# Softmax totals inverted by chunk and applied to x1 where the networks load it

## The reference, cut to what matters

```python
# attention: B=2, C=128, 12288 queries and 768 keys per batch
kv_pool = kv.reshape(B, H//4, 4, W//4, 4, C).mean(axis=(2, 4))
k = v = kv_pool.reshape(B, -1, C) @ w_sr
s = (q @ k.transpose(0, 2, 1)) / np.sqrt(C)
s = s - s.max(-1, keepdims=True)
a = np.exp(s)
a /= a.sum(-1, keepdims=True) + 1e-09
x1 = (a @ v).reshape(B * N, C)
# first network, d_ff = 2048
h = x1 @ moe_w_in
x2 = (h * np.cos(h)) @ moe_w_out
# second network
h = x2 @ moe2_w_in
out = (h / (1 + np.exp(-1.702 * h))) @ moe2_w_out
```

## Time and profile before

| | |
|---|---|
| median of 3 runs | 2651.97 us |
| span of the profiled execution, first to last instruction | 2650.0 us |
| PE busy | 2642.2 us (100%) |
| DVE busy | 2174.3 us (82%) |
| ACT busy | 1929.0 us (73%) |
| POOL busy | 2038.4 us (77%) |
| attention, joining stretch, networks | to about 554 us, to about 600 us, to 2650.0 us |

### The profile page before, as it was taken

The page is one execution under the profiler, slowest core; times in us unless marked ns, Lnnn a source line. Parts: engine busy times, 40 slices in busy tenths (PEclk is TensorE's granted clock), DMA queues, the critical chain, the costliest instruction groups (busy, mean ns, idle before and its releaser), DMA issues.

```text
span 2650.0 us, 40918 instructions
## 1 busy us (share of the span) xinstructions
PE 2642.2 (100%) x12551; PEld 2213.6 (84%) x12551; DVE 2174.3 (82%) x2786; ACT 1929.0 (73%) x2502; POOL 2038.4 (77%) x1900
## 2 busy tenths in 40 slices
PE   9999999999999999999999999999999999999999
PEld 8888888888888888888888888888888888888887
DVE  8999899987778787878787878787888888787876
ACT  5777777787777777777777777777777777777776
POOL 4887677579787878888878787878887878787873
PEclk9999999999999999999999999999999999999999
DMA  7323222200000000000000000000000000000000
GB/s 204 72 48 97 61 48 48 52 21 13 8 16 8 16 9 15 15 9 16 8 16 8 16 8 16 8 16 8 16 8 16 8 16 8 16 8 16 11 10 13
DMA packets 217397, 67.66 MB, mean 26 GB/s; under 512 B 200336, under 2 KB 201488, under 8 KB 216336
## 3 DMA queue, kind: packets, MB, share of 16 engines
q1 hardware_dynamic: 216304, 67.07, 11.0%
q10 hardware_dynamic: 1056, 0.13, 0.0%
HBM read 42.01 MB, written 25.17 MB: 25 GB/s over the span
## 4 chain that ended last, share of the span: by engine, by line
PE 99%; DVE 0%; DMA 0%; ACT 0%; SPq 0%; issue 0%
PE psum L644 29%; PE psum L645 29%; PE psum L646 29%; PE psum L691 7%; PE psum L848 5%; DMA kv_all<-in_kv 0%; PE psum L746 0%; DVE kv_all L1136 0%; DVE g_lo L1308 0%; PE psum L728 0%; PE psum L762 0%; PE psum L661 0%; DVE kv_all L1139 0%; PE psum L668 0%; ACT g_hi L1078 0%; PE psum L735 0%
## 5 line engine op out<-in xcount | busy, mean ns | idle before, releaser
L629 POOL TENSOR_TENSOR g_lo<-g,g_hi 128x512 fp32r<-128x512 f32 x768 | 1132.8, 1475 | 62.3 <-ACT g_hi L1085 2.2
L1308 DVE TENSOR_TENSOR g_lo<-g,g_hi 128x1024 fp32r<-128x1024 f32 (+1 forms) x396 | 666.8, 1685 | 413.9 <-ACT g L1080 413.9
L1078 ACT ACTIVATE g_hi<-psum 128x1024 fp32r<-128x1024 f32 (+1 forms) x396 | 397.3, 1003 | 557.3 <-PE psum L646 557.3
L626 POOL CAST g_hi<-g 128x512 fp32r<-128x512 f32 x750 | 503.8, 672 | 341.7 <-DVE g L1299 341.7
L644 PE MATMUL psum<-x_hi,w_lo 128*128 128x512 f32 x1536 | 597.9, 389 | 0.0
L644 PE MATMUL psum<-g_hi,w_lo 128*128 128x512 f32 x1536 | 597.7, 389 | 0.1
L646 PE MATMUL psum<-x_hi,w_hi 128*128 128x512 f32 x1536 | 597.6, 389 | 0.0
L645 PE MATMUL psum<-x_lo,w_hi 128*128 128x512 f32 x1536 | 597.5, 389 | 0.0
L646 PE MATMUL psum<-g_hi,w_hi 128*128 128x512 f32 x1536 | 597.5, 389 | 0.0
L645 PE MATMUL psum<-g_lo,w_hi 128*128 128x512 f32 x1536 | 597.5, 389 | 0.0
L1299 DVE TENSOR_TENSOR g<-psum,g 128x512 f32<-128x512 f32 x768 | 489.7, 676 | 1.9 <-ACT g L1071 1.8
(11 more groups left out here) (104 smaller groups left out, 2779.0 us busy)
## 6 DMA issues: line engine op xcount, KB each, us to landing
x_dram<-x_out SPq DMA_DIRECT2D x48, 256.0 KB, 2.0
x_raw<-x_dram SPq DMA_DIRECT2D x48, 256.0 KB, 2.7
out<-y_blocks SPq DMA_DIRECT2D x190, 64.0 KB, 2.3
q_blocks<-in_q SPq DMA_DIRECT2D x184, 64.0 KB, 2.2
kv_all<-in_kv SPq DMA_DIRECT2D x6, 1024.0 KB, 9.7
kv_all<-in_kv SPq DMA_DIRECT2D x4, 1536.0 KB, 12.0
w_raw<-in_moe_w_in SPq DMA_DIRECT2D x2, 1024.0 KB, 4.9
q_blocks<-in_q SPq DMA_DIRECT2D x2, 256.0 KB, 5.1
```

Of the source, the lines that this page charges most:

```text
L626: nc.gpsimd.tensor_copy(g1_hi[at][:, t], g1[at][:, t]).then_inc(g1_hi_ready, 1)
L629: nc.gpsimd.tensor_tensor(g1_lo[at][:, t], g1[at][:, t], g1_hi[at][:, t].bitcast(F32), ALU.subtract).then_inc(g1_lo_ready, 1)
L1078: nc.scalar.activation(g2_hi[ring2(j, p)][:, t], h2[buffer2(j)][:, t], ACT.Silu, scale=GELU)
L1308: nc.vector.tensor_tensor(g2_lo[ring2(j, p)][:, t], g2[ring2(j, p)][:, t], g2_hi[ring2(j, p)][:, t].bitcast(F32), ALU.subtract).then_inc(g ...
```

## The change

`scale` on POOL, `invert_total` on DVE and the one scaling of the first subtile on DVE go. The exponentials write their totals into eight columns, two chunks of four. Once a chunk, at the third subtile, DVE adds 1e-9 to four totals and inverts them (`invert_totals`), and SP saves the four columns to `inverse_dram` (`save_inverse`), 512 numbers of four bytes that go from 128 partitions to token order. PE waits for `exp_done` where it waited for `probs_ready`. x1 is stored unnormalised. `load_x1` issues a second DMA, which copies the chunk's 512 inverses to all 128 partitions (`x1_inv`), and `round_x1` on POOL multiplies x1 by them before it rounds it. POOL's remaining work in the attention is no longer tied to steps: folds, `unscale_piece` and `split_piece` run one behind another as soon as their data is there, the splits after `values_summed` has reached 24.

```diff
+            def save_inverse(c, n):
+                sp.wait_ge(inverse_ready, c + 1)
+                sp.dma_start(inverse_dram[c].rearrange("(j p) -> p j", p=P),
+                             inverse[:, n * SUB:(n + 1) * SUB],
+                             allow_slow_non_contiguous=True).then_inc(inverse_saved[n], 16)
...
             def load_x1(c, n):
                 sp.dma_start(x1_raw[n][:, :], x1_dram[c]).then_inc(x1_loaded[n], 16)
+                sp.dma_start(x1_inv[n][:, :],
+                             inverse_dram[c].rearrange("(o n) -> o n", o=1).to_broadcast([P, TOK])
+                             ).then_inc(x1_loaded[n], 16)
...
             with sp.Fori(0, 6) as r:
                 for n in range(2):
                     load_queries(r * 2 + (n + 10), n)
+                    save_inverse(r * 2 + (n + 7), 1 - n)
                     save_x1(r * 2 + (n + 5), 1 - n)
...
             for c in range(2):
                 sp.wait_ge(x1_saved[c], 16)
+                sp.wait_ge(inverse_saved[c], 16)
                 load_x1(c, c)
             for c in range(CHUNKS - 5, CHUNKS):
                 save_x1(c, c % 2)
+                if c + 2 < CHUNKS:
+                    save_inverse(c + 2, c % 2)
...
             def round_x1(c, n, loads):
-                pool.wait_ge(x1_loaded[n], 16 * loads)
+                pool.wait_ge(x1_loaded[n], 32 * loads)
+                nc.gpsimd.tensor_tensor(x1_raw[n][:, :], x1_raw[n][:, :], x1_inv[n][:, :],
+                                        ALU.mult).then_inc(x1_scaled, 1)
+                pool.wait_ge(x1_scaled, c + 1)
                 pool.sem_inc(x1_taken, 1)
                 nc.gpsimd.tensor_copy(x1_hi[n][:, :], x1_raw[n][:, :]).then_inc(x1_hi_ready, 1)
...
-            for s in range(FIRST_SPLIT):
-                if s > 0:
-                    scale(s, s % ROUND)
-                if s == SUB + 1:
-                    lower_queries(0)
...
+            lower_queries(0)
+            for s in range(UNITS * FOLDS):
+                fold(*divmod(s, FOLDS))
+            pool.wait_ge(unscale_made, 1)
+            pool.wait_ge(raw_loaded[3], 16)
+            for m in range(F // WP_COLS):
+                unscale_piece(m)
...
+            pool.wait_ge(values_summed, CB)
+            with pool.Fori(0, WEIGHT_PIECES // SUB) as r:
+                for p in range(2 * SUB):
+                    split_piece(r * SUB + p // 2, p % 2)
+            for c in range(2):
+                round_x1(c, c, 1)
...
-                    pe.wait_ge(probs_ready, s + (b * SB + 1))
+                    pe.wait_ge(exp_done, s + (b * SB + 1))
...
+            def invert_totals(c, n, saves):
+                cols = slice(n * SUB, (n + 1) * SUB)
+                dve.wait_ge(exp_done, c * SUB + SUB)
+                nc.vector.tensor_scalar(total[:, cols], total[:, cols], 1e-9, None,
                                         ALU.add).then_inc(total_guarded, 1)
+                if saves is not None:
+                    dve.wait_ge(inverse_saved[n], saves * 16)
+                dve.wait_ge(total_guarded, c + 1)
+                nc.vector.reciprocal(inverse[:, cols], total[:, cols]).then_inc(inverse_ready, 1)
...
-            invert_total(0, 0)
-            dve.wait_ge(inverse_ready, 1)
-            nc.vector.tensor_scalar(probs[0][:, :], probs[0][:, :], inverse[:, 0:1], None,
-                                    ALU.mult).then_inc(probs_ready, 1)
-            invert_total(1, 1)
...
-                        invert_total(s + (b * SB + 1), (j + 1) % SUB)
...
+                    if j == SUB - 2:
+                        invert_totals(c + b * CB, p // SUB, None if b == 0 and static and c < 2
+                                      else r + b * CB // 2)
```

More of the change, by code:

```diff
@@ L180, in attention_and_networks @@
     neg_max = put("neg_max", [P, SUB], F32)
-    total = put("total", [P, SUB], F32)
-    inverse = put("inverse", [P, SUB], F32)
+    total = put("total", [P, 2 * SUB], F32)
+    inverse = put("inverse", [P, 2 * SUB], F32)
     max_parts = put("max_parts", [P, 2], F32)
@@ L203, in attention_and_networks @@
     probs_t_odd = [None, put_probs_t("_odd1")]
+    x1_inv = [put(f"x1_inv{n}", [P, TOK], F32) for n in range(2)]
     place[0] = w_lo_at + 4 * F
@@ L241, in attention_and_networks @@
     x1_dram = nc.dram_tensor("x1_dram", (CHUNKS, P, TOK), F32, kind="Internal").ap()
+    inverse_dram = nc.dram_tensor("inverse_dram", (CHUNKS, TOK), F32, kind="Internal").ap()
     psum = nc.alloc_psum_tensor("psum", [P, 8 * BANK], F32)
@@ L324, in attention_and_networks @@
     inverse_ready = sem("inverse_ready")
-    probs_ready = sem("probs_ready")
+    inverse_saved = [sem(f"inverse_saved{n}") for n in range(2)]
+    x1_scaled = sem("x1_scaled")
     probs_transposed = sem("probs_transposed")
@@ L451, in _ @@
             load_queries(3, 1)
+            save_inverse(0, 0)
             load_windows(2)
@@ L454, in _ @@
                 load_queries(c, c % 2)
+                save_inverse(c - 3, (c - 3) % 2)
                 if c >= 5:
@@ L469, in _ @@
                     load_queries(r * 2 + (n + 26), n)
+                    save_inverse(r * 2 + (n + 23), 1 - n)
                     save_x1(r * 2 + (n + 21), 1 - n)
@@ L492, in _ @@
                 sp.wait_ge(x1_saved[n], 16 * (CHUNKS // 2))
+                sp.wait_ge(inverse_saved[n], 16 * (CHUNKS // 2))
             for c in range(2):
@@ L969, in split_queries, with exponentials @@
                                      scale=SCALE).then_inc(q_hi_ready, 1)
-            def exponentials(s, s4, n):
+            def exponentials(s, s4, n, at):
                 act.wait_ge(max_ready, s + 1)
@@ L974, in exponentials @@
                                      bias=neg_max[:, s4:s4 + 1],
-                                     accum_out=total[:, s4:s4 + 1]).then_inc(exp_done, 1)
+                                     accum_out=total[:, at:at + 1]).then_inc(exp_done, 1)
             def store_x1(c, n, n_saved, src=x1_ps):
@@ L1018, in _ @@
             round_keys(3)
-            exponentials(0, 0, 0)
-            exponentials(1, 1, 1)
+            exponentials(0, 0, 0, 0)
+            exponentials(1, 1, 1, 1)
             round_values(3)
@@ L1054, in _ @@
                     if not (final and static and s + 2 >= SB):
-                        exponentials(s + (b * SB + 2), (j + 2) % SUB, (p + 2) % 4)
+                        exponentials(s + (b * SB + 2), (j + 2) % SUB, (p + 2) % 4, (p + 2) % ROUND)
                     if j == 2 and not (final and static and c + 2 >= CB) and not (
@@ L1255, in _ @@
                                                      (p - 1) // SUB))
-                    if not (final and static and s + 1 >= SB) and not (b == 0 and static and s == 0):
-                        if b == 0 and static and s == 1:
-                            split_values(3)
-                        invert_total(s + (b * SB + 1), (j + 1) % SUB)
+                    if b == 0 and static and s == 1:
+                        split_values(3)
                     if b == 0 and static and s == 1:
```

14 lines of the change are left out of this document (removed).

## The result

| | before | after |
|---|---|---|
| median of 4 executions each, us | 2651.93 (2651.87 to 2652.02) | 2697.65 (2692.15 to 2701.85) |
| ratio, 95% interval | | 1.0171 [1.0157, 1.0185] |
| profiled span, us | 2650.0 | 2694.0 |
| first and last of ACT's copies of a finished x1 to `x_out`, start us | 46.38, 561.29 | 46.59, 604.13 |
| POOL busy, us | 2038.4 | 1853.8 |

The change costs 46 us; the forecast was 2652.3 us. Of the 44.0 us by which the profiled span grew, 42.6 lie between the first and the last of the copies to `x_out`, that is in the attention; the networks take what they took.

A forecast was written before the change was run, and what follows sets the result against it. PE's own matmuls were taken to bound the kernel except at the start and the joining stretch. Span 2650.0 - 0.7 (start) + 1.0 (joining) = 2650.3 us, with the median 1.97 us above it: 2652.3 us, range 2649.8 to 2656.5.

The forecast's parts named there:

- The step that failed: Attention, SP: the added save of inverses, SP busy 2.8 to 7.2 us of 10.95 a chunk, hides; 0 us.
- Rival (e): Attention: the 4-byte save blocks SP from about 8.6 us an issue; at 12 us it costs 156 us, 2808; chance 0.02.
- a query load is used two chunks after it is issued: Attention, SP: the next query load starts some 1 us later behind the save of inverses, which hides; 0 us.
- The start: To about 50 us: DVE without inversions shortens PE's waits, -0.7 us; ends 0 (DVE held up by POOL's folds) and -1.3.
- since that step loses its own pair, it grows by nothing: Attention, DVE: one pair of small operations a chunk, in the step that also transposes queries, adds no time.
- the going of POOL's scaling is worth nothing: Attention, 60 to 554 us: removing POOL's scalings (280.5 us) gains nothing, since PE's own matmuls are late next.
- Rival (a): Attention: POOL's traffic sets PE's pace, so its going gives back 4.8 us (2647.5) or 13 us (2639); chance 0.03.
- The joining stretch: 566 to 600 us: POOL's multiplication in `round_x1(2)` delays pair 10's halves and PE; net +1.0 us, ends +0.3 and +2.3.
- (c): Joining stretch: the delay grows as pairs 11 and 12 fall behind as well, 2 x 1.4 us, 2655; chance 0.10.
- (d): Joining stretch: POOL's multiplication finds its gap, leaving only the gain at the start, 2651.3; chance 0.12.
- The networks: 46 steady chunks: the added multiplication on POOL, 1.39 us, at most 2.25, is absorbed; 0, chunks stay at 43.52 us.
- rival (b): Networks: DVE loses its slack to POOL in every chunk and PE stalls, 46 x 0.54 = 25 us, 2677; chance 0.05.

The follow-up runs named there:

- spread4: Kernel after, with each of a save's 512 four-byte pieces in 64 bytes of its own in memory (output not the reference's): 2652.51 us.
- p16_late: Kernel after, saving 128 pieces of 16 bytes, POOL reading `x1_inv` with a step of four, and `round_x1(2)` moved behind pair 11: 2651.8 us.
- rows2: Against rows: DVE's transposition of the inverses one step later, in a chunk's fourth step, and `round_x1(2)` behind pair 11: 2651.54 us.
- p16: Kernel after, saving 128 pieces of 16 bytes, with POOL reading `x1_inv` with a step of four: 2653.07 us, span 2651.0 us.
- rows: Kernel after, with inverses turned by a 32x32 block transpose on DVE and saved as 16 pieces of 128 bytes in four DMAs: 2661.85 us.
- onecol: Kernel after, saving one of the four columns, 128 four-byte pieces side by side (output not the reference's): 2663.46 us.
- b_save: Kernel before, plus 45 saves of 512 four-byte pieces of a constant tile that nobody reads: 2766.18 us.

## Why the prediction was wrong

**The step that failed** is "The save's price is not in the trace: 512 pieces of 4 bytes. The nearest row is a query load (a quarter of 1.92 us to issue), the far end is the slowest issue in the trace, 4.87 us. ... Both hide; I take 0." The two rows are prices of SP's time to issue, and by that measure the step was right: 0.41 us in most chunks, never over 4.76. But a DMA has a second price, the time in which it holds up what stands behind it, and neither row bounds that. It measured 8 to 10 us a save, in front of the query loads and the save of x1, and about 45 us in all (2697.65 against the 2652.51 of spread4). Rival (e), with 0.02, had the right culprit and the wrong place: it made the save's own issue the thing that blocks, set its threshold at 8.6 us an issue and gave 2808 us. That issue stayed at a twentieth of the threshold in most chunks, and the loss came anyway; where SP was held, at the start and at the weights, it was held in the query loads behind the save.

The sentence "a query load is used two chunks after it is issued" is the second half of the failure. That slack covers a load of 10 us in a steady chunk, but not where the loads have just begun (60 us) nor where weights are loaded between them (297 us), and it covers no hand-over between engines that comes late; there was no term for any of the three.

The Trainium skill's page "DMA: Bandwidth & Descriptors" (Specifications) says that a transfer below 512 bytes is a read-modify-write. That would have been a ground to doubt the 0. It doesn't tell the cases here apart, though: pieces of 4, 16 and 128 bytes all lie below it, and only the four-byte pieces that share 16 bytes cost 12 us and more. One reading that would fit the runs is that neighbours which rewrite the same bytes must go one after another, but no run shows it; the runs show only which layouts are slow, and the cause inside the DMA stays open.

**The start:** 0.7 us of gain were forecast. The two waits went much as worked out. In DVE's rows `q_lo` starts at 29.15 and not 29.39, PE's stall for it falls from 0.62 to 0.24 us, and the one of the earlier trace rows is gone; by 40 us the kernel after is 0.6 us ahead if its start, 0.16 later, is allowed for. Then it gives most of this back. DVE, and PE behind it:

```profile
42.84 0.73 DVE L1230 TENSOR_SCALAR total<-total 128x4 f32<-128x4 f32 x1
43.60 0.18 DVE L1235 RECIPROCAL inverse<-total 128x4 f32<-128x4 f32 x1
43.70 0.99 DVE L1199 TENSOR_TENSOR probs_t_lo_odd<-psum,probs_t_hi_odd 128x384 fp32r<-128x384 f32 x2
```

```profile
44.37 0.92 PE L855 MATMUL psum<-ident,probs 128*128 128x128 f32 x6 [0.65 <-DVE probs_t_lo_odd L1199]
```

The addition of 128x4 takes 0.73 us here, beside POOL's folds, and 0.167 on average over its 48. "since that step loses its own pair, it grows by nothing" was short by this. It is nearly the end that the prediction named for the start, "0 (DVE held up by POOL's folds, which now start at about 38 us instead of 60)": the first copy to `x_out` is at 46.59 against 46.38, and in spread4 at 46.30.

**The attention from 60 us on:** that the going of POOL's scaling is worth nothing is shown by p16_late and rows2, with chunks of 10.93 to 10.95 us and no change in time. Rival (a) is out with them.

**The joining stretch:** right in mechanism and place, and nearly in size. POOL, then PE, of the kernel after:

```profile
630.30 1.30 POOL L598 TENSOR_TENSOR x_raw<-x_raw,x_inv 128x512 f32<-128x512 f32 x1
631.77 0.61 POOL L602 CAST x_hi<-x_raw 128x512 fp32r<-128x512 f32 x1 [0.17 <-POOL x_raw L598]
632.34 2.53 POOL L636 TENSOR_TENSOR g_lo<-g,g_hi 128x512 fp32r<-128x512 f32 x2
```

```profile
633.68 0.50 PE L651 MATMUL psum<-g_hi,w_lo 128*128 128x512 f32 x1 [0.53 <-POOL g_lo L636]
...
634.92 0.50 PE L651 MATMUL psum<-g_hi,w_lo 128*128 128x512 f32 x1 [0.28 <-POOL g_lo L636]
```

The two stalls stand at the two halves of pair 10, where the earlier trace rows had put them; the hand-over from multiplication to cast took 0.17 us where the prediction had 0.08. Taking `round_x1(2)` away from there gave 1.27 us, against 1.0 forecast. Rivals (c) and (d) are out.

**The networks:** 43.52 us a chunk, as before. POOL's multiplication takes 1.90 us on average (91.2 us over 48), inside the 1.29 to 2.15 of the estimate; rival (b) didn't come about. Apart from the slow save the sum was off by the 0.7 us between p16's span and the forecast's, about the size of the gain at the start that was given back.

**What rows and rows2 showed was in the trace of before as well.** DVE is busy 92 of 100 us there, but its slack in the step that transposes queries was worked out nowhere. In rows one more small operation in that step cost 10 us, by the same gap in the working that missed the 0.65 us at 44.37.

## What to carry to other kernels

Price a DMA twice: what it takes to issue, and how long it keeps the DMA engines from whatever is next in its queue and in the others. A small transfer whose pieces lie side by side at four bytes each is the one to distrust; take it for nothing only with a landing time of the same layout in hand, and else give a partition's values one run of 16 bytes or spread them. And when a busy engine loses one operation and gains another, work out its slack in that very step, since 0.2 us a chunk comes back as 10 us.

## What the runs showed of the hardware

- A store of four-byte pieces from 128 partitions to neighbouring addresses in memory held up the query loads behind it until 8 to 10 us after their issue with 512 pieces (kernel after), and 8.4 us with 128 (onecol), instead of 2.2. With 16 bytes a piece, or 16 bytes of room for each, the store landed in 1.4 to 3.0 us; with 64 bytes of room, in 1.9 us.
- The slow pieces don't look slow themselves: their packets last 9.9 ns on average in the record. It shows on the packets behind them (74.7 ns instead of 12.5), on the DMA row (0.9 to 1.0) and on loads that land late.
- In the kernels with the slow save DVE and ACT heard of PE's ends late, though neither has to do with the DMA: in the 12 "remote" waits of the kernel after PE's semaphore updates are recorded 1.5 to 2.8 us after the matmul's end, in b_save up to 4.5 us, in spread4 and the kernel before there is none. POOL's hand-overs to itself stayed on time meanwhile (0.16 us). What held the updates stays open.
- In PE's stalls of 6.8 us (to 62.12) and 3.6 us (to 298.35) the granted clock fell to the lower of its two levels, 1.2 instead of 2.4 GHz, and stayed there from 58.6 to 65.4 us and from 297.5 to 304.3; six transpositions took 1.54 and 1.51 us there instead of 0.82.
